# Two layers' output products regrouped over pairs of steps in a fused three-stage kernel

## The reference

```python
out = np.einsum('hk,bskhg->bshg', w, x_unf)          # 7 taps, softmaxed weights per head
x = out.reshape(B * S, D)                            # 8192 x 192
h = x @ w_in;  g = h * (1 / (1 + np.exp(-1.702 * h)));  x = g @ w_out      # d_ff = 2048
h = x @ w_in2
P = a[0] + a[1] * h + a[2] * h**2 + a[3] * h**3
Q = 1 + abs(b[0]) * abs(h) + abs(b[1]) * h**2
out = (P / (Q + 1e-6)) @ w_out2
```

## Time and profile before

| what | value |
|---|---|
| median of 3 runs | 1321.98 us (1319.99 to 1322.09) |
| the profiled execution | 1322.17 us, of it span 1320.4 us |
| mean granted TensorE clock, share of full speed | 0.995 |
| PE busy | 1275.4 us (97%) |
| DVE busy | 1126.0 us (85%) |
| ACT busy | 1093.0 us (83%) |
| POOL busy | 533.4 us (40%) |
| PE idle before L358, for DVE's L811 | 12.7 us in all |

### The profile page before, as it was taken

One profiled execution on the slowest core, in us unless ns is written; L12 is line 12 of the kernel. 1 busy time (PEld: TensorE's weight loads), 2 busy tenths in 40 slices (PEclk: granted clock), 3 DMA queues, 4 the chain that ended last, 5 costly groups with the idle time before them and its releaser, 6 DMA issues. The chain is left out here.

```text
span 1320.4 us, 15207 instructions
## 1 busy us (share of the span) xinstructions
PE 1275.4 (97%) x5068; PEld 745.1 (56%) x5068; DVE 1126.0 (85%) x1231; ACT 1093.0 (83%) x1250; POOL 533.4 (40%) x383
## 2 busy tenths in 40 slices
PE   5999999999999999999999999999999999999786
PEld 3555656566565655656565565655556565565332
DVE  5768998989889898988989898897989889777886
ACT  5658888888888888888888888888888888888774
POOL 1414434444443444434444443444434444444221
PEclk9999999999999999999999999999999999999998
DMA  7324455545445454544545455454544545454000
GB/s 170 97 70 110 116 120 125 131 112 138 110 125 123 118 137 105 142 114 124 124 115 138 107 138 118 124 124 106 141 113 124 131 122 113 108 131 103 12 1 24
DMA packets 107822, 148.60 MB, mean 113 GB/s; under 512 B 20961, under 2 KB 45281, under 8 KB 107745
## 3 DMA queue, kind: packets, MB, share of 16 engines
q0 software_dynamic: 33984, 61.88, 27.5%
q1 hardware_dynamic: 73284, 85.75, 19.3%
q10 hardware_dynamic: 477, 0.01, 0.0%
HBM read 13.64 MB, written 6.29 MB: 15 GB/s over the span
## 5 line engine op out<-in xcount | busy, mean ns | idle before, releaser
L922 POOL TENSOR_TENSOR work<-work 128x1024 f32<-128x1024 f32 x127 | 305.0, 2402 | 529.7 <-ACT work L586 475.2
L928 POOL DMA_DIRECT2D g_low<-g_nhi x236 | 207.8, 1017 | 195.6 <-DMA g_low<-g 189.3
L358 PE MATMUL acc_b<-g,down 128*64 128x512 f32 x512 | 249.0, 609 | 12.8 <-DVE g L811 12.7
L338 PE MATMUL acc_a<-g,down 128*128 128x512 f32 x512 | 255.2, 621 | 0.0
L783 DVE TENSOR_TENSOR work<-work,h 128x1024 f32<-128x1024 f32 x128 | 156.3, 1221 | 112.0 <-ACT work L586 110.5
L358 PE MATMUL acc_b<-g,down_b 128*64 128x512 f32 x480 | 231.7, 605 | 0.0
L573 ACT ACTIVATE work<-h,par 128x1024 f32<-128x1024 f32 x128 | 142.5, 1113 | 96.4 <-PE h L332 93.0
L324 PE MATMUL h<-x_a_hi,up_a_hi 128*128 128x512 f32 x512 | 207.8, 406 | 13.2 <-DVE x_a_lo L814 5.5
L325 PE MATMUL h<-x_a_lo,up_a_hi 128*128 128x512 f32 x512 | 200.9, 392 | 0.0
L326 PE MATMUL h<-x_a_hi,up_a_lo 128*128 128x512 f32 x512 | 200.8, 392 | 0.0
L327 PE MATMUL h<-x_b,up_b_hi 128*128 128x512 f32 x512 | 200.4, 391 | 0.0
(11 more groups left out here) (123 smaller groups left out, 1935.9 us busy)
## 6 DMA issues: line engine op xcount, KB each, us to landing
g_low<-g SPq DMA_DIRECT2D x236, 256.0 KB, 2.4
g_low<-g_nhi POOLq DMA_DIRECT2D x236, 256.0 KB, 3.8
out<-y_out SPq DMA_DIRECT2D x15, 384.0 KB, 3.0
x_in<-in_x SPq DMA_DIRECT2D x16, 256.0 KB, 3.1
x_in<-in_x SPq DMA_DIRECT2D x32, 64.0 KB, 2.7
work<-in_moe_w_in SPq DMA_DIRECT2D x8, 256.0 KB, 4.3
work<-in_moe_w_in SPq DMA_DIRECT2D x16, 128.0 KB, 4.5
x_b<-x_hb SPq DMA_DIRECT2D x30, 64.0 KB, 2.1
```

The source lines that it names most:

```text
L338: done = mm(L2.acc_a[:], L2.down[:, f, 0:P], L2.g[:, slot, k, :], start=f == 0, stop=f == STEPS - 1)
L358: return mm(acc_b[l.acc_row:l.acc_row + DB, :], l.down_b[:, f, :], l.g[:, slot, k, :], start=f == 0, stop=f == STEPS - 1)
L922: tt(m, sq[v % 2], seed, ALU.mult).then_inc(m_ready, 1)
L928: pool.dma_start(g_low[:, n % 2, k, :], g_nhi[:, n % 2, k, :], accum_op=ALU.add)\
```

## The change

It leaves each product and its operands as they are and changes in which step they run.

- `down_b` for both layers runs in even steps only, for two duos each: layer 1's duos n-2 and n-1, layer 2's n-14 and n-13 (new `downs_b`).
- Layer 2's `down_a` runs in odd steps only, for its duos n-13 and n-12 (new `downs_a`). Layer 1's `down_a_parts` stays in each step.
- From n = 130 on each step takes one duo for both; step 130 takes three duos of `down_b`.
- `L2.g` has three buffers. The one semaphore of each `g` becomes two, one for each kind of product, and who writes the buffer waits for both.
- `S_ACC2` goes from 3 to 4, and ScalarE there copies `y_a` in the middle of its step and both halves of `y_b` at its end.
- VectorE's L775 waits for `g1_b_used` of 8*i duos in place of `acc1_b_done`.

```diff
-S_ACC2 = 3
+S_ACC2 = 4
@@
+        L1.g = sb("g1", [P, 2, 2, NT])
+        L2.g = sb("g2", [P, 3, 2, NT])
@@
+        def downs2_a(n):
+            if n >= TOTAL + 2:
+                pairs = [n - LAG_DOWN2]
+            else:
+                pairs = [n - LAG_DOWN2 - 1, n - LAG_DOWN2] if n % 2 else []
+            return [v for v in pairs if live(v)]
+        def downs2_b(n):
+            if n == TOTAL + 2:
+                pairs = [n - LAG_DOWN2 - 2, n - LAG_DOWN2 - 1, n - LAG_DOWN2]
+            elif n > TOTAL + 2:
+                pairs = [n - LAG_DOWN2]
+            else:
+                pairs = [n - LAG_DOWN2 - 2, n - LAG_DOWN2 - 1] if n % 2 == 0 else []
+            return [v for v in pairs if live(v)]
+        def downs1_b(n):
+            return [v for v in (n - LAG_DOWN1 - 1, n - LAG_DOWN1) if live(v) and n % 2 == 0]
@@
+            def downs_b(n):
+                duos1, duos2 = downs1_b(n), downs2_b(n)
+                for at in range(max(len(duos1), len(duos2))):
+                    v1 = duos1[at] if at < len(duos1) else -1
+                    v2 = duos2[at] if at < len(duos2) else -1
...
+                        if e2 == 0:
+                            wait(pe, acc2_b_read, 2 * (v2 // DUOS))
...
+                    for k in range(2):
+                        if live(v2):
+                            if last(v2):
+                                pe.wait_ge(last_g2, k + 1)
+                            done2 = down_b(L2, e2, v2 % 3, k)
+                        if live(v1):
+                            unit = down_b_apart if v1 < DUOS else down_b
+                            done1 = unit(L1, e1, v1 % 2, k)
+                    if live(v2):
+                        done2.then_inc(g2_b_used, 1)
+                    if live(v1):
+                        done1.then_inc(g1_b_used, 1)
+            def downs_a(n):
+                v1 = n - LAG_DOWN1
+                for v2 in downs2_a(n):
...
+                    down_a(v2).then_inc(g2_a_used, 1)
...
+                    down_a_parts(v1, v1 % 2).then_inc(g1_used, 1)
@@
-                downs(i, s, v1, v2)
+                downs_b(n)
+                downs_a(n)
@@
                     wait(act, g1_used, n - 1)
+                    wait(act, g1_b_used, n - 1)
@@
                 if s == S_ACC2 and 0 <= i - 2 < TILES - 1:
-                    act.wait_ge(acc2_b_done, i - 1)
+                    act.wait_ge(g2_a_used, DUOS * (i - 1))
                     wait(act, y_transposed, 2 * (i - 2))
-                    y_b_half(0)
+                    fn(y_a[:], L2.acc_a[:], ACT.Copy).then_inc(acc2_a_read, 1)
@@
                 if s == S_ACC2 and 0 <= i - 2 < TILES - 1:
+                    act.wait_ge(g2_b_used, DUOS * (i - 1))
+                    y_b_half(0)
                     y_b_half(1)
-                    act.wait_ge(g2_used, DUOS * (i - 1))
-                    fn(y_a[:], L2.acc_a[:], ACT.Copy).then_inc(acc2_a_read, 1)
@@
                 if s == S_X2 and tile_live(t):
-                    dve.wait_ge(acc1_b_done, t + 1)
+                    dve.wait_ge(g1_b_used, DUOS * i)
@@
-                    wait(dve, g2_used, v - 1)
+                    wait(dve, g2_a_used, v - 2)
+                    wait(dve, g2_b_used, v - 2)
                     stt(gv, s2, d2, zv, ALU.add, ALU.mult).then_inc(g2_ready, 1)
```

More of the change, by code:

```diff
@@ L332, in up_rest, with down_a @@
                 return mm(banks[:, k, :], up_b_lo[rows, f * P:(f + 1) * P], l.x_b[rows, p, :], start=False, stop=True)
-            def down_a(d, slot):
+            def down_a(v):
                 for k in range(2):
-                    f = 2 * d + k
-                    done = mm(L2.acc_a[:], L2.down[:, f, 0:P], L2.g[:, slot, k, :], start=f == 0, stop=f == STEPS - 1)
+                    f = 2 * (v % DUOS) + k
+                    done = mm(L2.acc_a[:], L2.down[:, f, 0:P], L2.g[:, v % 3, k, :], start=f == 0, stop=f == STEPS - 1)
                 return done
@@ new lines, in downs_a @@
+            def downs_a(n):
+                v1 = n - LAG_DOWN1
+                for v2 in downs2_a(n):
+                    if v2 == 0:
+                        pe.wait_ge(down2_loaded, 16 * CHUNKS)
+                    if v2 % DUOS == 0:
+                        wait(pe, acc2_a_read, v2 // DUOS)
+                    if last(v2):
+                        pe.wait_ge(last_g2, 2)
+                    else:
+                        pe.wait_ge(g2_ready, v2 + 1)
+                    down_a(v2).then_inc(g2_a_used, 1)
@@ L408, in downs @@
                 if live(v1):
+                    e1 = v1 % DUOS
                     if v1 < DUOS and e1 % 2 == 0:
@@ L413, in downs @@
                     if e1 == 0:
[L414 to L431, removed]
-                        done = unit(L1, e1, slot1, k)
-                        if e1 == DUOS - 1 and k == 1:
-                            done.then_inc(acc1_b_done, 1)
-                if live(v2):
-                    if e2 == 0:
-                        wait(pe, acc2_a_read, v2 // DUOS)
-                    down_a(e2, slot2).then_inc(g2_used, 1)
-                if live(v1):
-                    if e1 == 0:
-                        wait(pe, x2_hi_done, i)
-                        wait(pe, x2_lo_done, 2 * i)
-                    down_a_parts(v1, slot1).then_inc(g1_used, 1)
+                        wait(pe, x2_hi_done, v1 // DUOS)
+                        wait(pe, x2_lo_done, 2 * (v1 // DUOS))
+                    down_a_parts(v1, v1 % 2).then_inc(g1_used, 1)
             def step(i, s, p):
                 n = i * DUOS + s
-                u, v1, v2 = n - LAG_UP2, n - LAG_DOWN1, n - LAG_DOWN2
+                u = n - LAG_UP2
                 d2, p2 = u % DUOS, u // DUOS % 2
```

34 lines of the change are left out of this document (22 added, 12 removed).

## The result

| | us, median (lowest to highest) | ratio to before (95% interval) |
|---|---|---|
| before | 1321.97 (1319.99 to 1322.09) | |
| after | 1330.53 (1328.63 to 1331.78) | 1.0071 (1.0059 to 1.0084) |
| after, once more, beside 1320.82 | 1329.66 (1326.47 to 1330.65) | 1.0062 (1.0048 to 1.0076) |

The changed kernel is slower by 0.6 to 0.7%, 8 to 9 us. The forecast was 1325.8, slower by 3.8 us. The direction and the stated range (1320.8 to 1331.5) hold, the range by 1 us at its upper end: 1330.53 is beyond the 1323.5 to 1328.5 that the forecast gave itself, and stands where its third rival stood (1329 to 1332). The forecast is low by some 5 us, and the experiments find where they are.

What follows compares the result with a forecast made beforehand. TensorE's queue was taken as the bound up to step 127, the VectorE-ScalarE loop from 128. Terms -10.2 - 1.4 + 8.8 + 1.4 + 0.9 + 4.3 = +3.8 us gave 1325.8 us, range 1320.8 to 1331.5.

Steps and rivals of the forecast that it cites:

- third rival: VectorE's 9.47 us rule four steps per tile, losing both odd savings, with some g_low waits: 1329 to 1332 us; chance 0.15.
- Parts 1 and 2: TensorE's steps up to 127: each odd step saves 0.16 us by fewer shape changes, even steps nothing; 10.2 us less.
- fourth rival: The change doesn't shorten the odd step, as L332 drains longer into L338: 1336 us; chance 0.07.
- Part 3: TensorE's waits for layer 2's newest g before step 128 go; -1.4 us.
- part 4: Tile boundary, s = 0: L775 comes 1.71 us later and PE idles 0.63 us at 14 boundaries; +8.8 us.
- second rival: The tile boundary is free, with no wait and no lag: 1315.6 us, faster; chance 0.08.
- Late next: After each boundary, ScalarE and VectorE lag until s = 5: 0.1 us per boundary, +1.4 us; the gelu's wait costs nothing.
- Part 5: Step 128: L775 is 1.71 us late, VectorE regains 0.74, +0.9 us; nobody waits for step 130's additional passes.
- Part 6: Step 132: L358 waits for late y_b copies, PE idles about 7 us, then runs at half clock; +4.3 us (2.9 to 5).
- first rival: The end gives little: the late y_b copies cost 0 to 2.9 us, total 1321.5 to 1324.4; chance 0.25.

Runs made afterwards that it cites:

- Experiment 3: Changed kernel with one pair's products issued per step, as before, in the steps of s = 7 and s = 0; 1318.78 us, ratio 0.9977.
- Experiment 8: Kernel before with the down products taken as 64, 128, 64, 128 columns, two more changes of tile shape per step; 1371.96 us, ratio 1.0401.
- experiment 6: Kernel before with VectorE's x_b copies at s = 0 also waiting for layer 2's 128-column products of that step; 1348.82 us, ratio 1.0216.
- experiment 4: Changed kernel with only VectorE's x_b copies moved behind t3, TensorE unaltered; 1323.99 us, ratio 1.0023.
- experiments 1 and 5: Changed kernel with the last y_b and y_a copies at step 131: alone 1326.79 us, with x_b copies behind t3 1321.21, with the old boundary order 1316.62.
- experiment 2: Kernel before with the late y_b copies, and the y_a copy with them, made at step 132 instead of 131; 1326.92 us, ratio 1.0052.
- experiment 1: Changed kernel with the last y_b and y_a copies inside the loop made at step 131 again; 1326.79 us, ratio 1.0046.
- experiment 7: Kernel before with only VectorE's x_b copies moved behind t3; 1338.60 us, ratio 1.0135.
- experiments 9 and 10: Changed kernel with two buffers of layer 2's g, 1498.55 us; e8_bound_tail with only the 64-column products paired, 1393.95 us.
- e8_bound_tail: Changed kernel with the old order at s = 7 and s = 0 and the last y_b and y_a copies at step 131; 1316.62 us, ratio 0.9970.

## Why the prediction was right, point by point

**Parts 1 and 2, the odd steps.** Right in kind. Steps with s = 3 and 5 take 0.14 and 0.13 us less, s = 7 0.16, even steps are as before; 0.15 to 0.16 was said. Experiment 3 gives 0.13 to 0.14 undisturbed. Over 64 steps that is 8.6 us, not 10.2. Experiment 8 adds from the other side that a change costs 0.18 us. The fourth rival (no gain) is out. An estimate from the load alone, as the Trainium skill gives it ("TensorE: Matmul & The Clock Gate", LDWEIGHTS: columns over 1.2, in ns), would have been 0.05 us a step. The measured gain is over twice that.

**Part 3, the waits for g2.** The term was half right. Up to step 14, where 0.74 of its 1.4 us lay, the two traces of after are +0.3 and -0.5 us against before, where the sum had -1.9 with the odd steps: the time only moved between steps there. The waits for g in steps 45 and 82 of before (0.26 and 0.28 us, steps 0.7 us longer in all) are gone in after. What the later use of g is really worth I did not see: experiment 6, with a delay of 1.95 us in place of 1.74, shows that without it the late boundary would have cost some 0.8 us more in each tile (its 1.00 less the 0.21). It doesn't make the kernel faster, but it halves the price of part 4.

**Part 4, the boundary.** Right, to the figure: L817 at 4.39 us behind its L354 (3.8 to 4.4 said), the step longer by 0.64 (0.63 said), 14 times. The second rival (a free boundary) is out by experiment 3.

**Late next.** Right in size for the regular part, wrong in place, and too low in the sum. I had the 0.1 us per boundary as waits for t3 in s = 1 to 4 and had declared ScalarE's gelu free. Steps with s = 2 to 4 have no such loss. Instead the step with s = 1 keeps 0.07 of its 0.13 us, and experiment 4 has the gelu as its releaser. In after itself PE's load for layer 1's next hidden product waits 0.16 to 0.20 us for the gelu at s = 1 in each regular tile, and never in before. The prediction read right that L614 would start 1.6 us behind its L354, and that the lag stays until s = 5. The step that failed is the next one. It followed the lag along VectorE, and looked at what the gelu waits for (with a start 3.8 us behind L332, which is 3.62 in the trace), but not at who waits for the gelu: the banks that it reads and the transfers that it starts. The transfers of `g_low`, for which it kept up to 2 us in the range and none in the sum, took more. Five steps of after (20, 61, 67, 108, 124) are 0.5 to 1.1 us longer than their like, 3.4 us in all, and each has a PE row like this one:

```profile
577.54 0.50 PE L373 MATMUL acc_a<-g_nhi,down_nhi 128*128 128x512 f32 x1 [0.26 <-DMA g_low<-g_nhi]
```

Before has one such step (98), longer by 0.4. Of the 4.7 us missed in the middle these transfers are 2.9 (in the second trace 1.9 of 3.4); the largest part of the rest is the smaller odd saving (57 x 0.02 = 1.1). This is the third rival's "some waits for `g_low`" without its mechanism, as VectorE's pace took no odd saving from s = 2 on.

**Part 5.** Right: VectorE's g of step 128 stands 13.46 us behind that step's L354, where it was 12.54 behind L332, 0.92 later (0.9 said). That nobody waits for the passes added in step 130 holds only where PE comes through them early. In the second trace of after, with the lower clock in step 129, ScalarE's L614 waited 2.81 us for the hidden products behind them and VectorE lost 1.2 us; in the kernels with copies at step 131 ScalarE waits for a product behind them (experiments 1 and 5).

**Part 6, step 132.** Right, in mechanism and size: 7.13 us of waiting (about 7), then a stretch at half speed, and 4.5 to 4.7 us on VectorE (4.3 said, 2.9 to 5). Put alone into before it costs 5.2 to 5.4 (experiment 2). The first rival (0 to 2.9) is out; experiment 1 seemed to come near it only because its repair opens a wait of its own. That the whole end fits its 5.2 us (4.7 and 5.7) has luck in it. Up to VectorE's last g the two traces of after lose 6.0 and 7.4 us: part 5, part 6, and 0.4 and 2.1 us by the clock and the twelve passes. Behind that g they need 1.3 and 1.7 us less than before, whose last but one group of L358 ran at the lower clock (granted 0.52 in the mean):

```profile
1303.51 3.62 PE L358 MATMUL acc_b<-g,down 128*64 128x512 f32 x4 [2.71 <-DVE g L811]
```

In after the same group took 1.93 us at the upper level, behind 2.70 us of idle time. The end of the kernel has either form in both orders (1.93 us in experiment 7, which keeps before's order, and 3.37 in experiment 1, with after's), so this is chance too.

So the sum missed by 5 to 6 us in the traces: 1 to 2 at the start, where the removed wait and the odd steps were counted in full though other steps took them up, and 3 to 5 in the middle, of which two to three are transfers of `g_low`. The stated range held because its upper end reached into the third rival's times, not because the forecast's own terms add up to 1330.

## What to carry to other kernels

Pairing products to save changes of the tile's shape is worth what the trace says (0.14 us here), and it moves the last product of a group by whole passes. Look for who waits for that last product, and keep the old order in the one step where someone does: here that gave 0.9977 in place of 1.0066 (0.9970 with the copies at step 131). When a result comes late, follow it on every engine that reads it, and one step further: what that engine frees or sends late. Read the price of a wait from the engine that leads the stage: PE's rows in the last steps gave 3 us for what VectorE's rows show to be 5. And an order that uses a result later is worth something that shows only once the result is late; the same edit gained 5.7 us in one order and lost 17.8 in the other.

## What the runs showed of the hardware

The same program part can run at either clock level. This is the stretch from step 129's L354 to step 130's, in the two traces of after (us; busy time and instructions of PE, PEld, DVE, ACT and POOL; granted clock; DMA share; GB/s):

```profile
1238.40:1244.60 6.20, 6.20 (x19) 3.29 (x18) 4.42 (x5) 4.60 (x5) 0.17 (x1) 0.98 0.00 0
```
```profile
1235.00:1243.40 8.40, 8.40 (x19) 4.11 (x18) 5.53 (x6) 5.89 (x6) 0.50 (x2) 0.71 0.00 0
```

In both PE had stood idle for 6.4 us before step 129. In the first it was back at 2.4 GHz when this stretch began (granted clock 0.98), in the second it ran part of it at 1.2 GHz (0.71 in the mean): 2.2 us more for as many instructions. Of twelve traces with this part (all but those of experiments 9 and 10) five have the long form (8.4 to 8.9 us) and the others 6.1 to 6.6. Kernels whose instructions up to there are the same show both forms: before 6.27 and experiment 2's 8.90, experiment 3's 6.13 and e8_bound_tail's 8.49. PE's rows in one trace of the end are therefore uncertain by 2 us. On VectorE, which leads there, the g of step 129 stands 9.42 us behind that of 128 in before, 9.83 in after and 10.27 in its second trace.
